# Delta-rule attention and two feed-forward stages: the corner blocks of the triangular inverses formed ahead, in two bursts of small matmuls a tile

## The chip, the cores and the metric

The kernel runs on one core of a Trainium2 chip. Its engines are TensorE (PE, matmuls; PEld, its weight loads), VectorE (DVE), ScalarE (ACT), GpSimd (POOL) and SyncE (SP), which here issues most DMAs. They run side by side, each in its own program order, and wait for one another on semaphores. The metric is the device time of one execution in microseconds (us), lower is better.

## The reference

For each of 32 heads (4 batches of 8) and 768 steps, with keys k normalised over their 48 dimensions:

```python
y[t] = q[t] @ state
v_old = state.T @ k[t]
state = state + beta[t] * outer(k[t], v[t] - v_old)
```

The results of the heads, laid side by side, are x (3072 tokens by 384). Two feed-forward stages follow:

```python
h = max(x @ w_in, 0);  x = (h * h) @ w_out              # d_ff 2048
g = x @ w_gate;        out = (silu(g) * (x @ w_val)) @ w_out2   # d_ff 1536
```

## The kernel before

**Chunks and tiles.** The 768 steps are cut into 12 chunks of 64, n = 0 to 11. Two chunks make a tile, t = 0 to 5 ("tiles two to six" are t = 1 to 5); chunk n is half s = n mod 2 of tile t = n // 2. Inside a chunk the recurrence is a triangular system: the 64x64 inverse has two 32x32 blocks on its diagonal and one block under it. The stages of a chunk on PE are: G (gram matrix of the keys), KS (keys times state, taken from v to give `resid`), QK, U (inverse times `resid`), Z (gram times the first half of U), DZ (second diagonal inverse times Z, taken off `u_tok`), Y (result), DS (state update), X (transposes, four a tile, by both chunks). Z and DZ stand in for the missing block under the diagonal. Each of these, X apart, is a burst of 32 small fp32 matmuls (64 for Y); the trace counts two instructions for one fp32 matmul, so x64 for 32.

**Inverses.** The diagonal blocks of the gram matrices go to `tri_scratch` in memory, and come back as `tri`, one 32x32 block in each of 128 partitions. "lane" (one ACT step, five on DVE) makes the scales from norms and beta; then `solve` inverts all 128 blocks by 31 column steps of two instructions. POOL does this for t = 1 to 5 (line 644). The result `tinv` goes out to `inv_scratch` and is loaded back as the blocks of `inv` by eight DMAs (`load_blocks`, line 415). U waits for them.

**The feed-forward work around it.** The first stage is seven units u = 0 to 6 (the first tile in two halves, 256 tokens wide; the rest 512 wide). Unit u has steps f = 0 to 17; PE does nine up matmuls for f < 16, and nine down matmuls for f - 2. Slot 2f lies between the up and the down matmuls of step f, slot 2f + 1 behind the down ones. `plan(u)` names for each slot the attention stages that go there, and PE, ACT and DVE all follow it. For f >= 1, ACT and DVE also make `h_hi` and `h_lo` of step f - 1, which the down matmuls read; an engine held up in a slot holds these back too. In units 2 to 5 the attention stages are those of tile t = u, in units 0 and 1 those of chunks 1 to 3. Unit 6 and the second feed-forward stage have no attention work.

**Banks.** The attention stages take two of three PSUM banks in turn, so a stage waits until the stage before it (one bank) and the one before that (the other) have been copied out.

**SP's queue** is written out by hand, in order: a DMA whose semaphore isn't there yet holds back all behind it. `k_sq` (line 469) is a load for the key norms. ACT squares it in the stage "sq", and "sq" of chunk 4 stands in slot 24 of unit 0, in ACT's order before an `h_hi`.

Of the kernel before, what the change touches and what calls it, by code (L numbers as in the profile page):

```python
# [5 lines left out]
def program(nc, kt, qt, kz, ky, vy, beta, w1, w2, out):  # L6
# [27 lines left out]
    inv_dram = nc.dram_tensor("inv_scratch", (NIT, P, HALF * HALF), f32, kind="Internal").ap()  # L34
    x1_dram = nc.dram_tensor("x1_scratch", (KC, P, NIT * T), f32, kind="Internal").ap()

    ctx = ExitStack()
    with ctx:
# [35 lines left out]
        gram = [sb(att_mem, f"gram{i}", [P, 2, 8, C]) for i in range(GRAMS)]  # L74
        qk = sb(att_mem, "qk", [P, 2, 8, C])
        inv = [sb(att_mem, f"inv{s}", [P, 16, C]) for s in range(2)]
# [66 lines left out]
        inv_stored = sem("inv_stored")  # L143
        first_stored = [sem(f"first_stored{i}") for i in range(3)]
# [61 lines left out]
        def plan(u):  # L206
# [11 lines left out]
            if u == 0:  # L218
# [22 lines left out]
                put(26, "QK", 2)  # L241
                put(27, "lane", 2)
                put(28, "U", 2)
                put(30, "Z", 2)
                put(31, "root", 4)
                put(32, "DZ", 2)
            elif u == 1:
                put(1, "Y", 2)
                put(3, "DS", 2)
                put(3, "scale", 3)  # L250
                put(5, "KS", 3)
                put(6, "QK", 3)
# [8 lines left out]
            else:  # L261
                t, p = u, u + 1
                n0, n1, p0, p1 = 2 * t, 2 * t + 1, 2 * p, 2 * p + 1
                if t < NIT:
                    if p < NIT:
                        put(0, "G", p0)
                        put(10, "G", p1)
                        put(16, "lane", p)
                    put(2, "sq", n1)
                    put(4, "root", n1)  # L270
                    put(8, "scale", n1)
                    chain(n0, dict(KS=2, QK=4, U=5, Z=7, DZ=9, Y=11, DS=12))
                    chain(n1, dict(KS=14, QK=15, U=17, Z=19, DZ=21, Y=23, DS=24))
# [15 lines left out]
        MATMULS = ("G", "QK", "KS", "U", "Z", "DZ", "Y", "DS", "X")  # L289
# [21 lines left out]
        def emptied(stage_):  # L311
# [8 lines left out]
            if name == "U":  # L320
                return [(ready, n + 1) for ready in u1_ready]
            if name == "Z":
                return [(ready, n + 1) for ready in z_ready]
# [52 lines left out]

        FILLED = {"G": g_filled, "U": u1_filled, "Z": z_filled, "Y": y_filled}
# [34 lines left out]
        def load_blocks(eng, t, s, i):  # L412
            for ab in range(2):
# [3 lines left out]
                              ).then_inc(inv_loaded[s], 16)  # L417

# [24 lines left out]
        def _(sp):  # L443
# [49 lines left out]
            def load_inverses(t, s):  # L493
                sp.wait_ge(inv_stored, 16 * t)
                sp.wait_ge(dz_filled, 2 * t + s - 1)
                for i in range(2):
                    load_blocks(sp, t, s, i)
# [41 lines left out]
            load_inverses(1, 0)  # L539
            load_inverses(1, 1)  # L540
# [3 lines left out]
            store_both(5)  # L544
            load_triangles(2)
# [7 lines left out]
            load_k(4)  # L553
            load_q(4)
            load_ktok(4)
            store_inverses(2)
            load_inverses(2, 0)
            load_inverses(2, 1)

            for u in range(2, NIT):  # L560
                t, p = u, u + 1
                n1, n2 = 2 * t + 1, 2 * t + 2
                if p < NIT:
                    load_prep(2 * p + 1)
                    store_both(2 * p)
# [5 lines left out]
                if p < NIT:  # L571
                    if p < NIT - 1:
                        load_prep(2 * p + 2)
                    store_both(2 * p + 1)
                load_q(n1)
                if n1 < NCH - 1:
                    load_ktok(n1)
# [577 lines left out]
```

## Time and profile before

| | us |
|---|---|
| median of 3 runs | 1049.47 |
| lowest and highest | 1049.29, 1050.03 |
| the profiled execution | 1047.97 |
| its span, first to last instruction | 1046.3 |

| engine | busy us | share of the span |
|---|---|---|
| PE | 990.5 | 95% |
| DVE | 408.2 | 39% |
| ACT | 303.0 | 29% |
| POOL | 208.1 | 20% |

The span is one execution as the hardware profiler saw it. The sums below are made against the 1047.97 us of that same execution; what lies outside its span is 1.7 us. The median of the runs is 1.5 us above it. A start time in the rows is counted from the start of the span.

### The profile page before, as it was taken

The numbers are of one execution on the slowest core, as the hardware profiler recorded it, in microseconds if no ns is written. First come the engines' busy times: TensorE is split into PE (matmuls) and PEld (weight loads), VectorE is DVE, ScalarE is ACT, GpSimd is POOL, SyncE is SP. The second block draws the span as 40 slices with busy tenths as digits, with TensorE's granted clock in tenths as the row PEclk, the third lists the DMA queues.
The fourth block names the chain that finished last, engine by engine and source line by source line (L and its number), as shares of the span: only waits on it lengthen the run. The fifth ranks groups of instructions, "written<-read, shape, count | busy, mean of one in ns | idle before, by whom it ended". The sixth has DMA issues, their size and how long they took to land.

```text
span 1046.3 us, 24211 instructions
## 1 busy us (share of the span) xinstructions
PE 990.5 (95%) x10752; PEld 823.0 (79%) x10752; DVE 408.2 (39%) x693; ACT 303.0 (29%) x599; POOL 208.1 (20%) x337
## 2 busy tenths in 40 slices
PE   2189999999999999999999999999999999999998
PEld 2178899788778878878888888888888888888887
DVE  3965644434434434543256521322312311322222
ACT  2225333333323333332245411221212211212121
POOL 1186381028307703820000000000000000000000
PEclk9999999999999999999999999999999999999999
DMA  7656423431452052130044010100100100100000
GB/s 232 189 151 197 143 74 86 131 95 53 110 154 63 26 152 80 52 107 23 2 173 145 15 61 1 50 11 1 61 1 1 61 1 1 61 1 0 31 1 31
DMA packets 74392, 73.88 MB, mean 71 GB/s; under 512 B 53168, under 2 KB 53296, under 8 KB 74288
## 3 DMA queue, kind: packets, MB, share of 16 engines
q1 hardware_dynamic: 68624, 64.99, 21.0%
q10 hardware_dynamic: 5664, 7.34, 2.2%
q8 instruction: 85, 1.39, 0.6%
q14 instruction: 19, 0.16, 0.1%
HBM read 56.59 MB, written 15.73 MB: 69 GB/s over the span
## 4 chain that ended last, share of the span: by engine, by line
PE 83%; POOL 8%; DVE 3%; DMA 3%; issue 1%; SPq 1%; ACT 0%; ACTq 0%; POOLq 0%; DVEq 0%
PE bank L895 82%; POOL tinv L399 4%; POOL prod L396 4%; DVE first_tinv L399 1%; DVE first_prod L396 1%; SPq L415 1%; DMA k_sq<-in_ky 1%; DMA inv_scratch<-tinv 1%; POOL tri L390 0%; DMA k_dim<-in_kt 0%; DMA tri_scratch<-gram 0%; DMA first_tri<-tri_scratch 0%; DVE h_lo L856 0%; PE bank L1024 0%; DMA inv<-inv_scratch 0%
## 5 line engine op out<-in xcount | busy, mean ns | idle before, releaser
L895 PE MATMUL bank<-x_hi,w_hi 128*128 128x512 f32 (+1 forms) x768 | 295.3, 384 | 1.2 <-DVE x_lo L831 1.2
L895 PE MATMUL bank<-x_lo,w_hi 128*128 128x512 f32 (+1 forms) x768 | 289.6, 377 | 0.0
L895 PE MATMUL bank<-x_hi,w_lo 128*128 128x512 f32 (+1 forms) x768 | 289.4, 377 | 0.0
L895 PE MATMUL bank<-h_hi,w_hi 128*128 128x512 f32 (+1 forms) x552 | 210.7, 382 | 2.6 <-DVE h_lo L856 2.5
L895 PE MATMUL bank<-h_hi,w_lo 128*128 128x512 f32 (+1 forms) x552 | 204.8, 371 | 0.0
L895 PE MATMUL bank<-h_lo,w_hi 128*128 128x512 f32 (+1 forms) x552 | 204.8, 371 | 0.0
L874 DVE TENSOR_TENSOR stage<-bank,stage 128x512 f32<-128x512 f32 x72 | 49.8, 692 | 318.5 <-ACT stage L741 318.5
L895 PEld LDWEIGHTS bank<-x_hi,w_hi 128*128 128x128 f32 x768 | 145.2, 189 | 29.4 <-DVE x_lo L831 1.6
L895 PEld LDWEIGHTS bank<-x_hi,w_lo 128*128 128x128 f32 x768 | 145.2, 189 | 26.5
L895 PEld LDWEIGHTS bank<-x_lo,w_hi 128*128 128x128 f32 x768 | 145.4, 189 | 24.9
L850 DVE TENSOR_TENSOR stage<-stage,bank 128x512 f32<-128x512 f32 (+1 forms) x112 | 68.4, 611 | 224.3 <-ACT stage L715 224.2
L741 ACT ACTIVATE stage<-bank 128x512 f32<-128x512 f32 x72 | 43.1, 598 | 329.7 <-PE bank L895 329.7
L715 ACT ACTIVATE stage<-bank 128x512 f32<-128x512 f32 (+1 forms) x112 | 60.0, 536 | 226.8 <-PE bank L895 218.7
L895 PEld LDWEIGHTS bank<-h_hi,w_hi 128*128 128x128 f32 x552 | 103.8, 188 | 26.6 <-DVE h_lo L856 5.6
L895 PEld LDWEIGHTS bank<-h_hi,w_lo 128*128 128x128 f32 x552 | 103.9, 188 | 18.1
L895 PEld LDWEIGHTS bank<-h_lo,w_hi 128*128 128x128 f32 x552 | 104.0, 188 | 16.8
L649 ACT ACTIVATE h_hi<-stage 128x512 fp32r<-128x512 f32 (+1 forms) x184 | 108.2, 588 | 6.9 <-PE bank L895 6.9
L399 POOL TENSOR_TENSOR tinv<-tinv,prod 128x31 f32<-128x31 f32 (+15 forms) x155 | 96.0, 619 | 12.1
L396 POOL TENSOR_TENSOR prod<-tri,tinv 128x31 f32<-128x31 f32 (+15 forms) x155 | 88.3, 570 | 12.2
L856 DVE TENSOR_TENSOR h_lo<-stage,h_hi 128x512 fp32r<-128x512 f32 (+1 forms) x112 | 76.3, 682 | 21.7 <-ACT h_hi L649 21.4
L390 POOL TENSOR_TENSOR tri<-tri,lane_nw 128x1024 f32<-128x1024 f32 x5 | 13.2, 2638 | 206.2 <-DVE lane_nw L795 206.2
L877 DVE TENSOR_TENSOR h_lo<-stage,h_hi 128x512 fp32r<-128x512 f32 x72 | 49.1, 682 | 5.1 <-ACT h_hi L649 5.1
(84 smaller groups left out, 576.6 us busy)
## 6 DMA issues: line engine op xcount, KB each, us to landing
w_raw<-in_w SPq DMA_DIRECT2D x12, 576.0 KB, 3.8
k_dim<-in_kt SPq DMA_DIRECT2D x12, 512.0 KB, 4.7
q_dim<-in_qt SPq DMA_DIRECT2D x12, 512.0 KB, 3.8
k_prep<-in_kt SPq DMA_DIRECT2D x10, 512.0 KB, 4.2
x1s<-in_w ACTq DMA_DIRECT2D x12, 384.0 KB, 4.7
k_sq<-in_ky SPq DMA_DIRECT2D x12, 384.0 KB, 3.7
v_tok<-in_vy SPq DMA_DIRECT2D x12, 384.0 KB, 4.0
x_scratch<-x1s SPq DMA_DIRECT2D x18, 256.0 KB, 3.1
```

Of the source, the lines that this page charges most:

```text
L390: then(eng.tensor_tensor(a[:, :, :], a[:, :, :], lane_nw[:, :].unsqueeze(1).to_broadcast([P, HALF, HALF]), ALU.mult))
L396: then(eng.tensor_tensor(share, a[:, j:j + 1, j + 1:HALF].to_broadcast(block), x[:, 0:j + 1, j:j + 1].to_broadcast(block), ALU.mult))
L399: then(eng.tensor_tensor(below, below, share, ALU.add))
L415: eng.dma_start(inv[s][ab * C + i * HALF:ab * C + (i + 1) * HALF, :, i * HALF:(i + 1) * HALF], inv_dram[t, at + ab:at + HALF:2, :].rearran ...
L649: return act.activation(dst, src, ACT.Copy)
L715: act.activation(stage[:, f % 2, 0:w], up_bank[f % 2][:, 0:w], ACT.Relu).then_inc(relu_done, 1)
L741: act.activation(stage[:, f % 2, :], gate_bank[f % 2][:, :], ACT.Silu).then_inc(silu_done, 1)
L850: dve.tensor_tensor(stage[:, f % 2, 0:w], stage[:, f % 2, 0:w], up_bank[f % 2][:, 0:w], ALU.mult).then_inc(square_done, 1)
L856: dve.tensor_tensor(h_lo[:, (f - 1) % 2, 0:w], stage[:, (f - 1) % 2, 0:w], h_hi[:, (f - 1) % 2, 0:w].bitcast(f32), ALU.subtract).then_inc( ...
L874: dve.tensor_tensor(slot, val_bank[f % 2][:, :], slot, ALU.mult).then_inc(hid_done, 1)
L877: dve.tensor_tensor(h_lo[:, (f - 1) % 2, :], stage[:, (f - 1) % 2, :], h_hi[:, (f - 1) % 2, :].bitcast(f32), ALU.subtract).then_inc(hid_lo ...
L895: return pe.matmul(dst, lhsT, rhs, start=start, stop=stop, **kw)
```

## The change

The inverse's block under the diagonal is now formed for tiles t = 1 to 5, by two bursts a tile on PE: N1 multiplies, for both chunks, the gram block with the first diagonal inverse, and N2 multiplies the second diagonal inverse with that, 64 matmuls of 32x32 with 32 columns in each. N1 is copied out (negated) into the free corner of the gram tile by two instructions on ACT and two on DVE, N2 into the free corner of `inv_both` by three on each. U then uses the full inverse, and Z and DZ are left out for chunks 2 to 11. N1 and N2 read the inverses from the gram tiles' unused corner; they are brought there by 12 new DMAs a tile (`load_cross`), 8 of which read a transposed copy, which POOL makes with one `tensor_copy` behind the solve and SP stores with two DMAs (`flip_scratch`). In the schedule G of a tile is taken two tiles ahead, in slots 9 and 14; "lane" moves to slot 1 of the unit before (slot 4 of unit 1 for t = 2, slot 6 of unit 2 for t = 3); N1 stands in slot 32 of the unit before (slot 26 of unit 0 for t = 1, slot 2 of unit 2 for t = 2), N2 in slot 4 of the tile's own unit (slot 28 of unit 0 for t = 1). SP's queue is rewritten to match.

```diff
@@ plan(u) @@
             if u == 0:
...
                 put(24, "sq", 4)
                 put(24, "KS", 2)
-                put(26, "QK", 2)
-                put(27, "lane", 2)
-                put(28, "U", 2)
-                put(30, "Z", 2)
+                put(26, "N1", 1)
+                put(28, "N2", 1)
+                put(30, "QK", 2)
                 put(31, "root", 4)
-                put(32, "DZ", 2)
+                put(32, "U", 2)
             elif u == 1:
                 put(1, "Y", 2)
                 put(3, "DS", 2)
                 put(3, "scale", 3)
+                put(4, "lane", 2)
                 put(5, "KS", 3)
                 put(6, "QK", 3)
                 put(8, "U", 3)
-                put(11, "Z", 3)
-                put(14, "DZ", 3)
-                put(16, "Y", 3)
-                put(18, "DS", 3)
+                put(10, "G", 6)
+                put(12, "Y", 3)
+                put(15, "DS", 3)
+                put(18, "G", 7)
...
                 if t < NIT:
+                    if t == 2:
+                        put(2, "N1", t)
                     if p < NIT:
-                        put(0, "G", p0)
-                        put(10, "G", p1)
-                        put(16, "lane", p)
+                        put(6 if t == 2 else 1, "lane", p)
+                        put(32, "N1", p)
+                    if t + 2 < NIT:
+                        put(9, "G", 2 * t + 4)
+                        put(14, "G", 2 * t + 5)
                     put(2, "sq", n1)
                     put(4, "root", n1)
+                    put(4, "N2", t)
                     put(8, "scale", n1)
-                    chain(n0, dict(KS=2, QK=4, U=5, Z=7, DZ=9, Y=11, DS=12))
-                    chain(n1, dict(KS=14, QK=15, U=17, Z=19, DZ=21, Y=23, DS=24))
+                    chain(n0, dict(KS=2, QK=5, U=7, Y=10, DS=12))
+                    chain(n1, dict(KS=15, QK=16, U=18, Y=21, DS=23))
@@ new copies out of PSUM and new loads @@
+        def take_whole(copy, stage_, ab):
...
+            for r in range(2):
+                copy(inv_both[early(ab), :, 12 * r:12 * r + 4, HALF:C], rows[0][:, :, r, :, :])
+            copy(inv_both[early(ab), :, 4:12, HALF:C], bank_rows(BANKS[stage_][1], ab)).then_inc(whole_ready[ab], 2)
...
+        def load_cross(eng, t, s):
+            block = gram[(2 * t + s) % GRAMS]
+            for bp in range(2):
+                at = lanes(s, 1) + bp * 16
+                eng.dma_start(block[bp * C + HALF:bp * C + C, :, :, HALF:C].rearrange("c r m i -> c (r m) i"),
+                              inv_dram[t, at:at + 16, :].rearrange("m (c i) -> c m i", i=HALF)
+                              ).then_inc(blocks_loaded[s], 16)
+            for x in range(2):
+                for r in range(2):
+                    at = lanes(s, 0) + (x ^ r) * 16 + 8 * r
+                    eng.dma_start(block[x * C:x * C + HALF, r, :, HALF:C],
+                                  flip_dram[t, at:at + 8, :].rearrange("m (i c) -> i m c", c=HALF)
+                                  ).then_inc(blocks_loaded[s], 16)
@@ SP, POOL, PE @@
             def load_triangles(t):
...
                     sp.wait_ge(sub_step, SUB * (t - 1))
+                    sp.wait_ge(flip_stored, 32 * (t - 1))
...
             def store_inverses(t):
...
+                sp.wait_ge(flipped, t)
+                for s in range(2):
+                    at = slice(lanes(s, 0), lanes(s, 0) + HALF)
+                    sp.dma_start(flip_dram[t, at, :], tri[at, :, :].rearrange("p s t -> p (s t)")
+                                 ).then_inc(flip_stored, 16)
...
             store_inverses(1)
             load_q(2)
-            load_inverses(1, 0)
-            load_inverses(1, 1)
+            load_inverses(1)
+            store_both(5)
+            load_triangles(2)
             load_prep(6)
             load_ktok(2)
             load_ky(4)
-            store_both(5)
-            load_triangles(2)
...
                 solve(pool, t, tri, tinv, prod, sub_step, SUB * (t - 1))
+                pool.tensor_copy(tri[:, :, :], tinv[:, :, :].rearrange("p c i -> p i c")).then_inc(flipped, 1)
...
+                elif name == "N1":
+                    for s in range(2):
+                        pe.wait_ge(blocks_loaded[s], 96 * n)
...
```

**SP, unit 0, from the storing of tile 1's inverses on.** `tri_scratch<-gram` are the stores of gram blocks, `k_sq<-in_ky` the load that ACT's "sq" reads. Before:

```order
L491 DMA inv_scratch<-tinv 128x1024
L459 DMA q_dim<-in_qt 128x1024
L415 DMA inv<-inv_scratch 32x16x32 x8
L447 DMA k_prep<-in_kt 128x1024
L464 DMA k_tok<-in_kz 128x768
L469 DMA k_sq<-in_ky 128x768
L407 DMA tri_scratch<-gram 32x16x32 x4
L487 DMA tri<-tri_scratch 128x1024
```

and now:

```order
L543 DMA inv_scratch<-tinv 128x1024
L547 DMA flip_scratch<-tri 32x1024 x2
L510 DMA q_dim<-in_qt 128x1024
L460 DMA gram<-inv_scratch 32x16x32 x2
L466 DMA gram<-flip_scratch 32x8x32 x4
L460 DMA gram<-inv_scratch 32x16x32 x2
L466 DMA gram<-flip_scratch 32x8x32 x4
L450 DMA inv_both<-inv_scratch 32x16x32 x8
L442 DMA tri_scratch<-gram 32x16x32 x4
L539 DMA tri<-tri_scratch 128x1024
L498 DMA k_prep<-in_kt 128x1024
L515 DMA k_tok<-in_kz 128x768
L520 DMA k_sq<-in_ky 128x768
```

Two stores and twelve loads are new ahead of the `k_sq` load, and the four gram stores with the `tri` load have moved from behind it to ahead of it.

**ACT, unit 0, steps 12 to 14.** `k_sq<-k_sq` is "sq" of chunk 4, in slot 24. Before:

```order
L715 ACTIVATE stage<-bank 128x256
L672 ACTIVATE k_sq<-k_sq 128x768
L649 ACTIVATE h_hi<-stage 128x256
L649 ACTIVATE w_hi<-x1s 128x768
L715 ACTIVATE stage<-bank 128x256
L649 ACTIVATE h_hi<-stage 128x256
L680 ACTIVATE lane_t<-tri 128x32
```

and now:

```order
L792 ACTIVATE stage<-bank 128x256
L749 ACTIVATE k_sq<-k_sq 128x768
L718 ACTIVATE h_hi<-stage 128x256
L718 ACTIVATE w_hi<-x1s 128x768
L792 ACTIVATE stage<-bank 128x256
L738 ACTIVATE gram<-bank 32x2x8x32 x2
L718 ACTIVATE h_hi<-stage 128x256
```

"sq" keeps its place; the copies of N1 are new behind it, and the lane step of tile 2 has left this stretch.

**PE, the beginning of unit 2, around slot 2** (`state,k_dim` is KS of chunk 4, `x_hi,w_hi` and the like are the up matmuls of the unit). Before:

```order
L895 MATMUL bank<-x_hi,w_lo 128x512
L895 MATMUL bank<-state,k_dim 64x48 x32
L895 MATMUL bank<-x_hi,w_hi 128x512
L895 MATMUL bank<-x_lo,w_hi 128x512
L895 MATMUL bank<-x_hi,w_lo 128x512
```

and now:

```order
L980 MATMUL bank<-x_hi,w_lo 128x512
L980 MATMUL bank<-gram 32x32 x64
L980 MATMUL bank<-state,k_dim 64x48 x32
L980 MATMUL bank<-x_hi,w_hi 128x512
L980 MATMUL bank<-x_lo,w_hi 128x512
```

N1 of tile 2 stands ahead of KS. The burst of G that stood one step earlier (slot 0) is gone from unit 2.

## Rows read from the trace of the kernel before

**Rows 1.** The page, the chain that ended last, by engine, as shares of the span

```profile
PE 83%; POOL 8%; DVE 3%; DMA 3%; issue 1%; SPq 1%; ACT 0%; ACTq 0%; POOLq 0%; DVEq 0%
```

**Rows 2.** Timeline of PE, unit 4: start us, duration us, engine, line, instruction

```profile
380.33 0.39 PE L895 MATMUL bank<-h_lo,w_hi 128*128 128x512 f32 x1
380.56 0.39 PE L895 MATMUL bank<-h_hi,w_lo 128*128 128x512 f32 x1
380.88 1.15 PE L895 MATMUL bank<-resid,inv 32*64 32x48 f32 x64
381.95 0.50 PE L895 MATMUL bank<-x_hi,w_hi 128*128 128x512 f32 x1
```

**Rows 3.** Timeline of PE, unit 4, around DS, whose weights have 48 columns

```profile
391.84 0.39 PE L895 MATMUL bank<-x_hi,w_lo 128*128 128x512 f32 x1
393.02 0.50 PE L895 MATMUL bank<-h_hi,w_hi 128*128 128x512 f32 x1
```

**Rows 4.** Timeline of PE around U of chunk 8, and at U of chunk 10

```profile
369.55 0.39 PE L895 MATMUL bank<-h_hi,w_lo 128*128 128x512 f32 x1
...
371.17 0.50 PE L895 MATMUL bank<-x_hi,w_hi 128*128 128x512 f32 x1
...
459.54 1.15 PE L895 MATMUL bank<-resid,inv 64*64 64x48 f32 x64 [0.77 <-DMA inv<-inv_scratch]
```

**Rows 5.** Timeline of the end of unit 3, ACT and DVE; a gram's two copies

```profile
353.89 0.62 ACT L649 ACTIVATE h_hi<-stage 128x512 fp32r<-128x512 f32 x1
...
361.03 1.08 ACT L649 ACTIVATE gram<-bank 128x512 f32<-128x512 f32 x2 [0.52 <-PE bank L895]
...
354.55 0.69 DVE L856 TENSOR_TENSOR h_lo<-stage,h_hi 128x512 fp32r<-128x512 f32 x1
```

**Rows 6.** Timeline of SP's queue, unit 0: start us, us spent issuing, DMA, count

```profile
96.36 0.34 SPq L491 DMA_DIRECT2D inv_scratch<-tinv  x1
...
99.28 6.10 SPq L415 DMA_DIRECT2D inv<-inv_scratch  x8
...
106.52 0.43 SPq L469 DMA_DIRECT2D k_sq<-in_ky  x1
107.05 2.93 SPq L407 DMA_DIRECT2D tri_scratch<-gram  x4
113.97 0.34 SPq L487 DMA_DIRECT2D tri<-tri_scratch  x1
```

**Rows 7.** Timeline of ACT, unit 0, slot 24; in brackets what it waited for

```profile
112.56 0.84 ACT L672 ACTIVATE k_sq<-k_sq 128x768 f32<-128x768 f32 x1 [2.39 <-DMA k_sq<-in_ky]
```

**Rows 8.** Timeline of PE, unit 0, the down matmuls behind slot 26

```profile
114.22 0.39 PE L895 MATMUL bank<-h_hi,w_hi 128*128 128x256 f32 x1 [0.20 <-DVE h_lo L856]
```

**Rows 9.** The DMAs that load the tile `inv` (line 415, 512 runs each)

```profile
DMA to landing us min/median/max: 1.9/2.4/5.1
```

**Rows 10.** Timeline of POOL, the solve of tile 2, first and last rows

```profile
119.06 2.38 POOL L390 TENSOR_TENSOR tri<-tri,lane_nw 128x1024 f32<-128x1024 f32 x1 [18.74 <-DVE lane_nw L795]
...
160.84 0.27 POOL L399 TENSOR_TENSOR tinv<-tinv,prod 128x31 f32<-128x31 f32 x1
164.01 0.96 POOL L642 MEMSET tinv<- 128x1024 f32 x1 [2.89 <-DMA inv_scratch<-tinv]
```

**Rows 11.** Timeline of DVE: first lane step of tile 2; squaring of step 2, unit 1

```profile
117.66 0.18 DVE L791 TENSOR_SCALAR lane_t<-lane_t 128x32 f32<-128x32 f32 x1 [0.36 <-ACT lane_t L680]
...
135.68 0.41 DVE L850 TENSOR_TENSOR stage<-stage,bank 128x256 f32<-128x256 f32 x1
```

**Rows 12.** Timeline of PE, unit 2, slot 2

```profile
182.98 1.15 PE L895 MATMUL bank<-state,k_dim 48*64 48x48 f32 x64
```

**Rows 13.** Timeline of PE, the first matmuls of unit 0

```profile
66.80 0.58 PE L895 MATMUL bank<-x_hi,w_hi 128*128 128x256 f32 x1 [1.17 <-DVE x_lo L831]
...
70.37 0.29 PE L895 MATMUL bank<-x_lo,w_hi 128*128 128x256 f32 x1
70.50 0.28 PE L895 MATMUL bank<-x_hi,w_lo 128*128 128x256 f32 x1
```

More of the change, by code:

```diff
@@ L73, in program @@
         q_dim = sb(att_mem, "q_dim", [P, 16, C])
-        gram = [sb(att_mem, f"gram{i}", [P, 2, 8, C]) for i in range(GRAMS)]
+        grams = [sb(att_mem, f"gram{i}", [P, 2, 2, 8, C]) for i in range(GRAMS // 2)]
+        gram = [grams[i // 2][:, i % 2, :, :, :] for i in range(GRAMS)]
         qk = sb(att_mem, "qk", [P, 2, 8, C])
-        inv = [sb(att_mem, f"inv{s}", [P, 16, C]) for s in range(2)]
+        inv_both = sb(att_mem, "inv_both", [P, 2, 16, C])
+        inv = [inv_both[:, s, :, :] for s in range(2)]
         tri = sb(att_mem, "tri", [P, HALF, HALF])
@@ L143, in program @@
         inv_stored = sem("inv_stored")
+        flipped = sem("flipped")
+        flip_stored = sem("flip_stored")
+        blocks_loaded = [sem(f"blocks_loaded{s}") for s in range(2)]
+        cross_filled = sem("cross_filled")
+        cross_ready = [sem(f"cross_ready{x}") for x in range(2)]
+        whole_filled = sem("whole_filled")
+        whole_ready = [sem(f"whole_ready{ab}") for ab in range(2)]
         first_stored = [sem(f"first_stored{i}") for i in range(3)]
@@ L321, in emptied @@
                 return [(ready, n + 1) for ready in u1_ready]
+            if name == "N1":
+                return [(ready, 2 * n) for ready in cross_ready]
+            if name == "N2":
+                return [(ready, 2 * n) for ready in whole_ready]
             if name == "Z":
@@ L577, in _ @@
                     load_ktok(n1)
+                if g < NIT:
+                    if g < NIT - 1:
+                        load_prep(2 * g + 2)
+                    store_both(2 * g + 1)
                 if p < NIT:
-                    load_triangles(p)
                     load_v(n2)
@@ L665, in run @@
                     store_triangles(act, n, 1)
+                elif name == "N1":
+                    act.wait_ge(cross_filled, n)
+                    for bp in range(2):
+                        act.activation(cross_rows(n, 0, bp), bank_rows(BANKS[stage_][bp], 0), ACT.Copy, scale=-1.0
+                                       ).then_inc(cross_ready[0], 1)
+                elif name == "N2":
+                    act.wait_ge(whole_filled, n)
+                    take_whole(copy, stage_, 0)
                 elif name == "fetch":
@@ L805, in run @@
                                           mask[:, :].unsqueeze(1).to_broadcast([P, 8, C]), ALU.mult).then_inc(qk_ready, 1)
+                elif name == "N2":
+                    dve.wait_ge(whole_filled, n)
+                    take_whole(copy, stage_, 1)
+                elif name == "N1":
+                    dve.wait_ge(cross_filled, n)
+                    for bp in range(2):
+                        dve.tensor_scalar(cross_rows(n, 1, bp), bank_rows(BANKS[stage_][bp], 1), -1.0, None, ALU.mult
+                                          ).then_inc(cross_ready[1], 1)
                 elif name == "KS":
@@ L901, in run, with u_whole @@
                 t, s = divmod(n, 2)
+                def u_whole():
+                    if t == 0:
+                        pe.wait_ge(u_ready, 2 * (n + 1))
+                    else:
+                        for ready in u1_ready:
+                            pe.wait_ge(ready, n + 1)
                 for one in sorted(BEFORE[stage_]):
@@ L938, in run @@
                     done.then_inc(ks_filled, 1)
+                elif name == "N1":
+                    for s in range(2):
+                        pe.wait_ge(blocks_loaded[s], 96 * n)
+                        block = gram[(2 * n + s) % GRAMS]
+                        for m in range(8):
+                            for r in range(2):
+                                for bp in range(2):
+                                    at = (8 * s + m) * HALF
+                                    done = mm(pair[bp][early(bp ^ r), at:at + HALF], block[late(bp), r, m, 0:HALF],
+                                              block[late(bp), r, m, HALF:C])
+                    done.then_inc(cross_filled, 1)
+                elif name == "N2":
+                    for ready in cross_ready:
+                        pe.wait_ge(ready, 2 * n)
+                    for s in range(2):
+                        block = gram[(2 * n + s) % GRAMS]
+                        for r in range(2):
+                            for a in range(4):
+                                for ab in range(2):
+                                    for x in range(2):
+                                        at = (8 * s + 4 * (x ^ r) + a) * HALF
+                                        done = mm(pair[x][early(ab), at:at + HALF], block[early(x), r, 2 * a + ab, HALF:C],
+                                                  block[early(x), r, 2 * a + ab, 0:HALF])
+                    done.then_inc(whole_filled, 1)
                 elif name == "U":
                     pe.wait_ge(inv_loaded[s], 64 * (t + 1))
+                    if t > 0:
+                        for ready in whole_ready:
+                            pe.wait_ge(ready, 2 * t)
                     if n == 0:
@@ L961, in run @@
                                     at = (4 * r + a) * D
-                                    done = mm(pair[bp][toks(ab), at:at + D], gram[n % GRAMS][early(bp), r, 2 * a + ab, :],
+                                    done = mm(pair[bp][late(ab), at:at + D],
+                                              gram[n % GRAMS][early(bp), r, 2 * a + ab, HALF:C],
                                               u_tok[early(bp), ab, 4 * r + a, :])
@@ L976, in run @@
                 elif name == "Y":
[L977 removed]
+                    u_whole()
                     pe.wait_ge(qk_ready, 2 * (n + 1))
```

52 lines of the change are left out of this document (33 added, 19 removed).

## The prediction, made before the changed kernel ran

> **What bounds the kernel now.** I read the chain that ended last first. PE has 83% of it and POOL 8% [rows 1], so the kernel is a stream of matmuls with a few places in which something else comes last. Next I read PE's timeline, to see what the small bursts take out of the stream, and then the queue of SP, ACT and POOL at the places where the chain leaves PE. There are two kinds of cost to tell apart. A burst displaces the big matmuls for as long as it runs. A wait costs what PE stands idle, and only where the waiting engine holds up a later matmul.
>
> In the steady part a 512-wide matmul starts every 0.23 us. Across a burst of 32 small matmuls the next start comes 1.39 us after the last one, so the burst takes 1.39 - 0.23 = 1.16 us [rows 2]. DS, whose weights are 48 columns wide and not 64, takes 393.02 - 391.84 - 0.23 = 0.95 us [rows 3]. PE waits hardly at all there: U of each tile's first chunk takes 1.39 us, 0.23 above the plain 1.16, since QK just before it must be copied out first; and U of chunk 10 waited 0.77 us for its inverse [rows 4].
>
> Unit 0 is different. ACT stood 2.39 us in slot 24, until the `k_sq` load had landed at 112.56 [rows 7]. That load was issued at 106.52, behind eight loads of inverses which in turn waited for the store issued at 96.36 [rows 6]. ACT's next instruction makes an `h_hi`, and 1.66 us after 112.56 PE goes on with the down matmuls that read it [rows 8]. So in the kernel before, SP's queue is already the last to arrive in this place, by a hair: anything put ahead of the `k_sq` load moves the end of the kernel.
>
> **The change, part by part.**
>
> Bursts taken out. Z and DZ go for ten chunks. Those of chunk 2 belong to unit 0 and are counted there; the 18 others are in the steady part: 18 x 1.16 = 20.9 us less.
>
> Bursts put in. N1 and N2 are 64 matmuls of 32x32 each, and the trace before has none of this shape. From 64 to 48 columns of weights a burst of 32 fell by 0.21 us, so at 32 columns it would be 0.74, and one of 64 matmuls at most 1.48. If 0.27 us of each burst is its start and end, and counted once, 1.2. If narrow weights gain nothing, 2 x 1.16 = 2.3. I take 1.45, near the slope of rows 2 and 3. For t = 2 to 5 that is 8 x 1.45 = 11.6 us more (9.6 to 18.6). The moved G bursts cost the same where they now stand: each slot has the up and the down matmuls of a step around it, and ACT's two copies of a gram (1.08 us, [rows 5]) are done within the nine matmuls (2.05 us) behind it.
>
> Waits that go. U now stands two slots behind QK, not one, which takes away 3 x 0.23 for chunks 4, 6 and 8; and the solve of tile 5 starts early in the unit, so the 0.77 goes too [rows 4]: 1.5 us less.
>
> The end of units 2, 3 and 4. N1 in slot 32 puts two copies on ACT, of the size of a gram's half, ahead of the last `h_hi`. After N1 ends: 1.08 for the copies, 0.62 for `h_hi`, 0.69 for `h_lo` [rows 5], together 2.4, while PE has nine down matmuls (2.05) before it needs that `h_lo`. About 0.4 us each, 3 x 0.4 = 1.2 us more (0 to 2.4).
>
> The steady part alone thus gains 20.9 + 1.5 - 11.6 - 1.2 = 9.6 us. N2's copies (three on each of ACT and DVE, some 1.5 us) hide behind the nine down matmuls in front of QK; were that cover gone they would cost up to 1.5 us a tile. SP, ACT and DVE otherwise have room. The work on PE is not where this change is decided.
>
> First wait, unit 0. The stage "sq" of chunk 4 still stands in slot 24. Ahead of its load SP now has: the wait for POOL's transposing copy, two stores, and the wait until they have landed. The copy has 1024 elements a partition, between a memset of 0.96 and a two-input multiply of 2.38 us of that size [rows 10]; I take 1.6. With the stores it starts the loads at about 101.2 and not 99.28: 1.9 us. Then twelve loads. The eight inverse loads took 6.10 us to issue [rows 6]; the twelve move as many 128-byte runs as eight did (4 of 512, 8 of 256). I take 5.5 us, of 3.8 to 9.1. Then the gram stores, the wait until they have landed, and the load of `tri`, which before stood behind: from 107.05 to 114.31 [rows 6], 7.3 us. The load itself took 6.0 us to land in heavy traffic; I take 5.0. Together 1.9 + 5.5 + 7.3 - 1.0 = 13.7 us later (8.7 to 20): ACT would stand in slot 24 for some 16 us. What is queued behind it is the `h_hi` of step 11 and everything after; PE gets through up matmuls 13 and N1, and then stands at the down matmuls of step 11 which started at 114.22 before [rows 8]. N1 of tile 1 is free, beneath that wait. The rest of unit 0 has N2, QK and U where it had U, Z and DZ: about 0.4 us less. So 13.3 us more. All else that this order delays (`k_tok`, `v_tok`) is needed later than it comes.
>
> Second wait, unit 2, slot 2. N1 of tile 2 waits for its blocks, and KS of chunk 4 and all of PE's stream stand behind it. The clock for both sides starts in unit 1, so the first wait shifts them alike; in times of the trace before: the square of step 2 ends at 136.1 [rows 11]; the five lane steps on DVE and POOL's start took 1.4 us (117.66 to 119.06, [rows 10, 11]): POOL begins at 137.5. A solve took 42.05 us (119.06 to 161.11, [rows 10]); this one runs later, beside wider work of DVE, so I take 43: 180.5. Copy 1.6, two stores and their landing 2.8, twelve loads 5.5, landing 2.2 (median 2.4, least 1.9, [rows 9]): 192.6, and the second half of N1 behind it 0.7: 193.3. Without a wait PE would reach N1 at 182.98 [rows 12] less the G burst that is gone from slot 0, 181.8, and end it at 183.3. The wait is 10.0 us (6 to 18). For tiles 3 to 5 there is none: from lane in slot 1 or 6 to N1 in slot 32 are 60 us and more against some 58, with tile 3, whose solve begins near slot 6 of unit 2, the nearest: its blocks come about 7 us early.
>
> The clock. After its long wait for the first inverse, PE began unit 0 with 17 matmuls from 66.80 to 70.37, one every 0.21 us, and from there on one starts every 0.12 to 0.13 [rows 13], although the granted clock is shown as 1.00 there; that is the step between 1.2 and 2.4 GHz, and those 17 at 0.21 in place of 0.12 cost 1.5 us. Both new waits are over 9 us long, and I charge each with that: 3.1 us (0 to 4). The Trainium skill (TensorE: Matmul & The Clock Gate, What's actually happening) says that an idle TensorE falls back to 1.2 GHz; rows 13 agree, and no row shows how a wait of 10 us in mid-stream fares.
>
> **Sum.** Against the profiled execution: 1047.97 - 9.6 + 13.3 + 10.0 + 3.1 = 1064.8. The median of the runs lies 1.5 us above that execution, so 1066.
>
> **The rivals.**
>
> One wait only. The second wait is the longer chain of estimates (solve, copy, loads). If tile 2's blocks come before PE does, 10.0 and 1.5 go: 1054.7. It needs a chain 10 us shorter than computed; the solve alone, which POOL does as before, is 42 of its 56. 0.08.
>
> Faster, by short exchange. The place is SP's queue in unit 0. If twelve loads and two stores are issued side by side with what is in flight, `k_sq` lands some 5.5 us late, not 13.7, and tile 2's blocks are there when N1 is reached. That gives 1047.97 - 9.6 + 5.1 + 1.5 + 1.5 = 1046.5. It decides for faster when both waits with their slow stretches come to less than 7.5 us. For it: one load alone takes 1.9 us at least to land [rows 9], and the 6.10 us for eight [rows 6] are a crowded stretch. Against it: 7.3 us of the delay were measured as they stand, in this queue. 0.08. As much gain from cheaper bursts is not to be had, since 8 bursts at 1.2 give only 2 us more.
>
> Dear bursts. The time of a small matmul may have a floor, so that 32 columns cost more than I think. In rows 2 an instruction takes 1.15 / 64 = 18 ns; at 25 ns N1 and N2 would be 3.2 us each, 14 us more in all: 1080. That is what a rule would give that the Trainium skill states (TensorE: Matmul & The Clock Gate, Wait — 56ns, not 53.3ns?): no start closer than about 25 ns to the last however few the columns. Rows 2 lie below it already, for bursts that alternate among four parts of the array, as N1 and N2 do. 0.04.
>
> **How the numbers follow.** Both waits and the gain as computed: 0.76, 1066, by itself 1056 to 1078. One wait: 0.08. Faster by short exchange: 0.08. Dear bursts: 0.04. In between, the waits short and the gain just eaten: 0.04. Lows of all terms together give 1048 - 13 + 8.3 + 6 + 1.5 = 1051, highs over 1085; the range 1053 to 1080 leaves out the fast case, the even case and the far tails, 2 in 10. The measurement tells 0.2% (2.1 us) from no change; so faster 0.08, same 0.04, slower 0.88.
>
> **What would show it.** In the profile after: ACT waiting in unit 0 for `k_sq` some 16 us instead of 2.39, with PE idle behind it for 12 or so; a row of PE in unit 2 with about 10 us of waiting for the `gram` loads ahead of a burst of 32x32; no Z and DZ from there on, bursts N1 and N2 of 1.2 to 1.5 us, and units 3 to 5 each shorter than before by roughly 2 us. The prediction is wrong if `k_sq` lands before 118 or tile 2's blocks come before PE needs them; its size is wrong first in the issue time of the twelve loads and in POOL's copy.

## The result, and the profile of the changed kernel

| | before | after |
|---|---|---|
| median of four runs, us | 1049.75 | 1070.7 |
| lowest and highest | 1049.29, 1050.25 | 1069.93, 1073.3 |
| the profiled execution | 1047.97 | 1070.59 |
| its span | 1046.3 | 1068.9 |

The changed kernel takes 1.0196 times as long (95% interval 1.018 to 1.0212). The prediction said 1066 (1053 to 1080).

First the page of the kernel after: the share of each engine in the chain that ended last, which answers to [rows 1], and the granted clock in 40 slices, which was 9 in each on the page of before.

```profile
PE 80%; POOL 8%; DVE 4%; DMA 3%; issue 2%; SPq 2%; ACT 1%; ACTq 0%; DVEq 0%; POOLq 0%
PEclk9679699799999999999999999999999999999999
```

PE's share fell by three points; DVE, SP's queue, ACT and "issue" (waits for nothing that the profile shows) rose by one each. The clock dips in slices 2, 3, 5 and 8. Slices 2 and 3 are not a difference between the kernels: there PE waits for the first inverses in both, and its bursts of 64 instructions take up to 1.99 us in both, where [rows 2] have 1.15, though the page of before shows 9. So that page doesn't show every slow stretch, and the rows' durations have to be read with it. New are slices 5 (106.9 to 133.6 us) and 8 (187 to 213.8 us). The list of PE's waits names both places (columns: total us, times, longest us):

```profile
PE bank L980 <- DVE h_lo L941: 16.9, 6, 13.2
PE bank L980 <- DMA gram<-flip_scratch: 9.8, 2, 6.5
PE bank L980 <- ACT inv_both L718: 2.1, 4, 0.6
PE bank L980 <- ACT gram L738: 1.5, 1, 1.5
```

Their rows on PE's and ACT's timelines (columns as in [rows 7] and [rows 8]):

```profile
125.59 0.84 ACT L749 ACTIVATE k_sq<-k_sq 128x768 f32<-128x768 f32 x1 [15.55 <-DMA k_sq<-in_ky]
127.25 0.58 PE L980 MATMUL bank<-h_hi,w_hi 128*128 128x256 f32 x1 [13.23 <-DVE h_lo L941]
205.62 1.08 PE L980 MATMUL bank<-gram 32*32 32x32 f32 x64 [6.54 <-DMA gram<-flip_scratch]
209.97 1.08 PE L980 MATMUL bank<-gram 32*32 32x32 f32 x64 [3.26 <-DMA gram<-flip_scratch]
212.50 1.96 PE L980 MATMUL bank<-state,k_dim 48*64 48x48 f32 x64 [1.46 <-ACT gram L738]
```

**First wait.** ACT stands 15.55 us for `k_sq` in slot 24 of unit 0 (2.39 before, [rows 7]). PE names DVE's `h_lo`, but DVE had waited for ACT's `h_hi`, and ACT for the load. PE's group begins at 127.25, where [rows 8] have 114.22: 13.03 us later. **Second wait.** In unit 2 both halves of N1 wait for their loads, 6.54 + 3.26 = 9.80 us, and KS behind them 1.46 more.

Where the 22.6 us (1068.9 - 1046.3) are, by the start of ACT's copy `x1s<-bank` at the end of each unit:

| unit | before | after | length before, after | change | the prediction's terms |
|---|---|---|---|---|---|
| 0 | 127.53 | 144.07 | | +16.54 | +14.8 |
| 1 | 177.66 | 195.01 | 50.13, 50.94 | +0.81 | 0 |
| 2 | 267.78 | 300.35 | 90.12, 105.34 | +15.22 | +11.4 |
| 3 | 357.87 | 388.82 | 90.09, 88.47 | -1.62 | -1.6 |
| 4 | 448.02 | 474.66 | 90.15, 85.84 | -4.31 | -3.9 |
| 5 | 535.02 | 557.62 | 87.00, 82.96 | -4.04 | -4.0 |

Behind unit 5 nothing differs (511.3 us in both). Units 3 to 5 gain what was worked out (9.97 us against 9.5); units 0 and 2 lose more than that, and unit 1 loses 0.8 where nothing was forecast.

SP's queue in unit 0, which answers to [rows 6]:

```profile
99.00 0.80 SPq L547 DMA_DIRECT2D flip_scratch<-tri  x2
101.92 0.85 SPq L460 DMA_DIRECT2D gram<-inv_scratch  x2
102.81 2.25 SPq L466 DMA_DIRECT2D gram<-flip_scratch  x4
109.36 4.35 SPq L450 DMA_DIRECT2D inv_both<-inv_scratch  x8
113.81 2.85 SPq L442 DMA_DIRECT2D tri_scratch<-gram  x4
118.10 0.34 SPq L539 DMA_DIRECT2D tri<-tri_scratch  x1
119.43 0.43 SPq L520 DMA_DIRECT2D k_sq<-in_ky  x1
```

The granted clock in stretches around the waits (columns: stretch, us, busy us of PE, PEld, DVE, ACT, POOL with their counts, granted clock, DMA share, GB/s):

```profile
127.00:136.00 9.00, 8.75 (x159) 8.47 (x160) 5.41 (x11) 3.79 (x10) 0.00 (x0) 0.50 0.01 2
136.00:144.00 8.00, 7.13 (x164) 6.50 (x164) 3.33 (x6) 2.08 (x6) 0.00 (x0) 0.97 0.40 116
205.00:218.50 13.50, 8.15 (x205) 6.58 (x205) 2.91 (x5) 2.31 (x4) 0.00 (x0) 0.51 0.77 181
218.50:222.00 3.50, 3.50 (x138) 2.76 (x137) 2.76 (x5) 1.80 (x6) 0.00 (x0) 1.00 0.12 36
```

After the first wait PE works for 9 us at the lower level (0.50, 1.2 GHz) before it has 2.4 GHz again.

### The profile page after: what moved, and what is told of

The parts are those of the page before. It is cut to its first block, busy times and chain, and to the rows that moved or that the text cites. A ratio compares the mean times of both kernels' runs of the same rounds, so it can differ in the third digit from the quotient of the medians.

```text
span 1068.9 us, 24285 instructions
## 1 busy us (share of the span) xinstructions
PE 984.3 (92%) x10752; PEld 819.8 (77%) x10752; DVE 413.4 (39%) x698; ACT 304.4 (28%) x604; POOL 215.7 (20%) x342
## 4 chain that ended last, share of the span: by engine, by line
PE 80%; POOL 8%; DVE 4%; DMA 3%; issue 2%; SPq 2%; ACT 1%; ACTq 0%; DVEq 0%; POOLq 0%
PE bank L980 79%; POOL tinv L434 4%; POOL prod L431 3%; DVE first_tinv L434 1%; DVE first_prod L431 1%; SPq L466 1%; DMA tri_scratch<-gram 1%; DMA k_sq<-in_ky 1%; DVE h_lo L941 1%; PE bank L1145 0%; DMA k_dim<-in_kt 0%; POOL tri L425 0%; SPq L460 0%; DMA flip_scratch<-tri 0%; DMA first_tri<-tri_scratch 0%
## 5 line engine op out<-in xcount | busy, mean ns | idle before, releaser
L434 POOL TENSOR_TENSOR tinv<-tinv,prod 128x31 f32<-128x31 f32 (+15 forms) x155 | 92.5, 597 | 12.1
```

The source lines that it names most:

```text
L434: then(eng.tensor_tensor(below, below, share, ALU.add))
```

## The experiments

The theory from here on: the steady gain is real, and the time is lost in two separate places, both in the order of SP's queue and both with a slow stretch of TensorE behind them. The rivals: the waits are one (take away the first, and the second grows), or the moved loads only pass the delay on.

**e1, the first wait alone.**

```diff
             load_q(2)
+            load_ky(4)
             load_inverses(1)
...
             load_ktok(2)
-            load_ky(4)
```

> The changed kernel with one line of SP's queue moved: the k_sq load of chunk 4 is issued before the twelve loads of tile 1's inverses, not behind them, the gram stores and the tri load. Theory (this load's place in the queue makes the first wait): ACT's wait in slot 24 falls from 15.6 us to under 2, PE's wait of 13.2 us behind it goes, and with it the stretch at half clock (3.6 us); the loads behind come about 3 us later, so N1 of tile 1 waits some 2 us instead. 1070.7 - 16.8 + 1.5 = about 1055 us; the wait in unit 2 stays at about 11 us. Rival (the exchange of the inverses as a whole is too long there, and N1, N2 or U of unit 0 wait in place of ACT): at least 1062.

1059.37 us, 1.0083 (1.0062 to 1.0104), between the theory's 1055 and the rival's 1062. ACT no longer waits, unit 0 ends at 135.99, and the second wait is as long as it was (6.50 + 2.94 + 1.46): the two are independent. But 11 us came back and not 15. One row of DVE, two of the queue and two of PE show the rest:

```profile
106.00 0.95 DVE L853 TENSOR_REDUCE norm<-k_sq 128x16 f32<-128x768 f32 x1
...
106.97 0.35 SPq L520 DMA_DIRECT2D k_sq<-in_ky  x1
107.42 2.08 SPq L460 DMA_DIRECT2D gram<-inv_scratch  x2
...
116.39 0.75 PE L980 MATMUL bank<-gram 32*32 32x32 f32 x64 [1.03 <-DMA gram<-flip_scratch]
123.28 0.37 PE L980 MATMUL bank<-h_hi,w_lo 128*128 128x256 f32 x1 [2.14 <-issue]
```

The `k_sq` load isn't free to go: its buffer is released by DVE's reduction of the chunk before, and the queue stands until 106.97. So the inverse loads start at 107.42 (101.92 in the kernel after), N1 waits 1.03 us, and N1 to U come late in unit 0. Then PE stands 2.14 us for nothing that the profile shows, and its granted clock is 0.50 from 124 to 132 us. How long that lasts isn't fixed: in e3, whose unit 0 has the same program, 15 matmuls of 256 columns are slow and not 24, and unit 0 ends 3.1 us earlier, at 132.85 (1 us of that is N1's wait, which isn't there).

**e4, the same cause in the kernel before.** Only `store_both(5)` and `load_triangles(2)` go ahead of the `k_prep`, `k_tok` and `k_sq` loads.

```diff
+            store_both(5)
+            load_triangles(2)
             load_prep(6)
             load_ktok(2)
             load_ky(4)
-            store_both(5)
-            load_triangles(2)
```

> The kernel before with only the order of SP's queue altered: the four gram stores and the tri load stand ahead of the k_prep, k_tok and k_sq loads, as in the changed kernel, with nothing else added. Theory: k_sq is issued some 7.1 us later (7.3 was my figure for this part of the delay), lands at about 119.6, and PE waits 7 us and then runs some microseconds at the slower clock: about 1059 us. Rival (the place was not critical, the wait is hidden): 1050.

1057.29 us, 1.0062 (1.0039 to 1.0085). The moved block by itself makes a wait of 7 of the 13 us, with nothing of N1 and N2 in the kernel:

```profile
121.19 0.58 PE L895 MATMUL bank<-h_hi,w_hi 128*128 128x256 f32 x1 [6.99 <-DVE h_lo L856]
120.00:124.00 4.00, 2.81 (x13) 2.81 (x14) 2.98 (x6) 2.14 (x6) 0.00 (x0) 0.50 0.03 10
```

A wait of 7 us is enough for the lower clock behind it, and shorter ones had it too (e1 above, e7 below). Unit 0 ends 8.6 us later.

**e2 and e3, the second wait alone, and both.** The attention stages of unit 2 go six slots later (N1 to slot 8). The grams of tile 4 stay in their slots, so that the first of them overwrites a gram tile before N2 has read it: the output isn't the reference's, the work is the same. SP stores and loads the inverses of tile 3 two loads earlier to suit (not shown).

```diff
+                    late = 6 if t == 2 else 0
                     if t == 2:
-                        put(2, "N1", t)
+                        put(2 + late, "N1", t)
...
-                    chain(n0, dict(KS=2, QK=5, U=7, Y=10, DS=12))
...
+                    chain(n0, dict(KS=2 + late, QK=5 + late, U=7 + late, Y=10 + late, DS=12 + late))
...
```

> The changed kernel with the attention stages of unit 2 (N1, KS, N2, QK, U, Y, DS of tile 2 and the scale step) six slots later, and the inverses of tile 3 stored and loaded two loads earlier in SP's queue to suit. Nothing is added or left out. Theory (N1 of tile 2 stands there too early for a solve that began in unit 1): its waits of 6.5 and 3.3 us, most of the 1.5 us of KS behind it and the slow clock after them (some 2.6 us) go: 1070.7 - 13 = about 1058, with the first wait unchanged. Rival (the lateness moves on to tile 3, whose solve starts in the same unit, or the later stages crowd the unit's end): 1064 or more.

1070.85 us, 1.0191 (1.0174 to 1.0207): no gain at all, as the rival had it. The wait is still 9.83 us, but it has another cause now:

```profile
215.37 0.26 ACT L762 ACTIVATE lane_t<-tri 128x32 f32<-128x32 f32 x1 [9.40 <-DMA tri<-tri_scratch]
220.46 1.96 PE L985 MATMUL bank<-state,k_dim 48*64 48x48 f32 x64 [9.83 <-DVE gram L894]
```

"lane" of tile 3 stands in slot 6 of this unit, and its load of `tri` is in SP's queue behind the 20 inverse loads of tile 2; the copies of N1, which free KS's bank, come only behind that step. In the kernel after, this hides beneath N1's wait. Both mended at once leave this one too:

> Both edits of the two runs before, together. Theory: the two waits are independent, so their prices add: 1070.7 - 16 - 13 = about 1042, below the kernel before (1049.7), since the steady part of the change gains 9 to 10 us. Rival (they share a cause, or the first hides part of the second): 1047 or more.

1058.2 us, 1.0067 (1.0049 to 1.0086), far from the theory's 1042, with 10.40 us of waiting in the same place (here too the gram is overwritten early).

**e5 and e6, the second wait and what hid behind it.** N1 of tile 2 in slot 8, its later stages and the grams of tile 4 behind, and the `tri` load of tile 3 ahead of the inverse loads (those of tile 3 two loads earlier, as in e2, not shown):

```diff
             store_inverses(2)
+            load_triangles(3)
             load_inverses(2)
-            load_triangles(3)
...
+                        put(16 if t == 2 else 9, "G", 2 * t + 4)
+                        put(20 if t == 2 else 14, "G", 2 * t + 5)
...
+                        chain(n0, dict(KS=9, QK=12, U=14, Y=17, DS=19))
+                        chain(n1, dict(KS=22, QK=23, U=25, Y=27, DS=29))
```

> The second wait again, after the run in which moving the stages of unit 2 left 9.8 us of waiting: there ACT and DVE stood in slot 6 for the lane step of tile 3, since the tri load stood behind the twenty loads of tile 2. Now the stages of tile 2 are six to seven slots later (KS one slot behind N1), the grams of tile 4 stand behind N2, and the tri load of tile 3 is issued ahead of the twenty loads. First wait left as it is. Theory (tile 2's exchange is late for everything that hangs on it, N1 and the tri load alike; both must be covered): unit 2 falls from 105.3 us to about 91, so 1070.7 - 14.5 = about 1056. Rival (the length of unit 2 comes from something else, or the crowded end of the unit gives it back): 1062 or more.

1056.2 us, 1.0055 (1.004 to 1.007). Unit 2 takes 90.25 us and not 105.34, no row waits for a gram load, and the first wait stays (13.79). With the `k_sq` load ahead as well:

> The same edit together with the k_sq load ahead of tile 1's exchange. Theory: prices add, 1059.4 - 14.5 = about 1045, faster than before by 0.4%. Rival (a shared cause): 1052 or more.

1043.69 us, 0.9933 (0.9919 to 0.9948): faster than the kernel before.

**e9, the last small wait.** After N2, QK waits for N2's copies:

```profile
222.52 1.16 PE L980 MATMUL bank<-q_dim,k_dim 48*64 48x64 f32 x64 [0.48 <-ACT inv_both L718]
310.41 1.10 ACT L718 ACTIVATE inv_both<-bank 32x256 f32<-32x256 f32 x3
310.29 1.36 DVE L837 COPY inv_both<-bank 32x256 f32<-32x256 f32 x3
```

e9 is e6 with QK, U, Y and DS of the first chunk one slot later in units 3 to 5.

```diff
-                        chain(n0, dict(KS=2, QK=5, U=7, Y=10, DS=12))
+                        chain(n0, dict(KS=2, QK=6, U=8, Y=11, DS=13))
```

> The kernel with the k_sq load first and tile 2 later, with QK, U, Y and DS of the first chunk of tiles 3 to 5 one slot further on, so that QK stands two groups of nine matmuls behind N2 and not one. Theory (QK waits 0.63, 0.63 and 0.34 us in that kernel's trace for the copies of N2, a wait that I had called hidden): 1.6 us less, 1043.7 to about 1042. Rival (the later stages wait instead): 1043.7 or more. The difference is near what a measurement can tell, so the waits in the trace decide.

1041.43 us (1039.24 to 1041.98), 0.9903 (0.9881 to 0.9925). The waits are gone, and units 3 to 5 take 87.77, 85.14 and 82.44 us (88.48, 85.87, 82.90 without this edit). It is the fastest version of the study.

**e7, the bursts for t = 2 to 5 only.** Units 0 and 1 are left as in the kernel before (with Z and DZ for tile 1's chunks) but for the two grams that go ahead. QK, U, Y and DS of each tile's first chunk are one slot later, as in e9.

```diff
-                put(26, "N1", 1)
-                put(28, "N2", 1)
-                put(30, "QK", 2)
+                put(26, "QK", 2)
+                put(27, "lane", 2)
+                put(28, "U", 2)
+                put(30, "Z", 2)
...
-                        put(2, "N1", t)
+                        put(0, "N1", t)
```

> The new blocks only for tiles 2 to 5 (t counted from 0); tile 1 keeps Z and DZ, its unit 0 and SP's order there are those of the kernel before, so the solve of tile 2 starts there as before and its blocks are in place before unit 2. N1 of tile 2 in slot 0 of unit 2, QK of a tile's first chunk one slot further from N2. Theory (the bursts are worth their price, only the two exchanges of the early tiles are late): bursts 16 x 1.16 off, 8 x 1.3 on, the U waits 1.5 off, 1.2 on at the unit ends: 1049.7 - 8.5 = about 1041 us, unit 0 as before at 127.5 us, no row of PE waiting for gram loads. Rival (the new bursts, copies and loads cost elsewhere what they save): 1048 or more.

1043.66 us, 0.994 (0.9923 to 0.9956). Tile 2's blocks come in time even for slot 0 of unit 2, since "lane" of tile 2 stands in slot 27 of unit 0 here. The median is 2.7 us above what was expected. The trace is of the fastest of the four executions (1040.69), so it can't show where the others lost that. What it does show is a unit 0 that ends 1.9 us later than before (129.43): SP's queue is 2.8 us later at the `k_sq` load (109.30 against 106.52, [rows 6]), ACT stands 4.45 us, PE 2.25 us, and the clock reads 0.62 for the 4 us behind that.

**e10 and e11, the reordering alone, and in e7.** The kernel before with the `k_sq` load first, and e7 with the same edit:

```diff
+            load_ky(4)
             load_inverses(1, 0)
             load_inverses(1, 1)
...
-            load_ky(4)
```

> The kernel before, with one edit: the load of chunk 4's k_sq goes ahead of the eight inverse loads of tile 1, so that ACT no longer stands in slot 24 of unit 0. It asks how much of the best version's gain is this reordering alone and has nothing to do with N1 and N2. Theory (the gain is mainly the bursts taken out): ACT's 2.39 us wait goes, PE gains at most the 1.7 us for which it stood behind it, and U of chunk 2 gets its inverse about 0.5 us later: 1048.5 us, within 0.2% of the kernel before. Rival (the queue's order was the whole gain): 1042 or less.

> The version in which only tiles three to six are changed (units 0 and 1 as before but for two grams), plus the load of k_sq ahead of the inverse loads. In that version ACT stood 4.45 us for k_sq in unit 0, and the granted clock went to 0.62 for the 4 us behind it; unit 0 ended at 129.43. If that wait is what is left of unit 0's loss, unit 0 ends near 127.5 and the time is 1041 to 1041.5 us, even with the best version (1041.4). Rival: the inverse loads behind it come late for U of chunk 2 and give it back: 1043.5, as without the edit.

1059.16 us, 1.0075 (1.0054 to 1.0096), and 1048.03 us, 0.997 (0.9958 to 0.9982). Both theories and both rivals missed. The same edit that gave 11 us after the change costs 8.6 before it (e10):

```profile
106.97 0.33 SPq L469 DMA_DIRECT2D k_sq<-in_ky  x1
107.41 5.03 SPq L415 DMA_DIRECT2D inv<-inv_scratch  x8
113.54 2.15 SPq L407 DMA_DIRECT2D tri_scratch<-gram  x4
121.19 0.34 SPq L487 DMA_DIRECT2D tri<-tri_scratch  x1
...
124.41 0.26 ACT L680 ACTIVATE lane_t<-tri 128x32 f32<-128x32 f32 x1 [9.03 <-DMA tri<-tri_scratch]
```

The load waits in the queue for DVE's reduction, all behind it moves back, and the `tri` load, issued at 113.97 in [rows 6], goes out at 121.19. "lane" of tile 2 stands in slot 27 of unit 0 in both versions, and ACT waits there for the load, 9.03 us and 8.81 us. Two things differ in the changed kernel, where the same edit pays: "lane" is in slot 4 of unit 1, and the wait that the edit takes away is 15.55 us and not 2.39. No run separates them. So the gain of the fastest version is not that of the reordering alone.

**e8, the price of the clock.** The kernel after with N1 of tile 1 run ten times, so that PE has work through most of the first wait.

```diff
-                    for s in range(2):
+                    for s in [0, 1] * (10 if n == 1 else 1):
                         pe.wait_ge(blocks_loaded[s], 96 * n)
```

> The changed kernel, in which PE runs the N1 burst of tile 1 ten times in place of once (each writes the same values), so that it is busy through nearly all of the 13 us in which ACT waits for the k_sq load. The wait itself stays. Theory (the slow stretch behind the first wait, 127.3 to 136.4 us at a granted clock of 0.50, comes from PE standing idle before it): the clock stays at 1.00 and the 3.6 us it cost come back: about 1067. Rival (small 32x32 matmuls don't count as work for the clock, or the clock falls for another reason): 1070.7, the same granted clock behind the wait as before. Rival 2 (the copies behind a longer burst come late): 1073.

1093.59 us, 1.0399 (1.0373 to 1.0424): every expectation missed, since the filling itself outlasted the wait.

```profile
117.52 1.50 PE L980 MATMUL bank<-gram 32*32 32x32 f32 x128 [2.20 <-issue]
137.53 1.93 PE L980 MATMUL bank<-gram 32*32 32x32 f32 x128 [1.52 <-issue]
140.00:144.00 4.00, 1.93 (x128) 1.79 (x128) 0.00 (x0) 0.00 (x0) 0.00 (x0) 0.50 0.01 4
```

A repeat takes at least 1.93 + 1.52 = 3.45 us, nearly half of it a wait for nothing shown. The clock reads 1.00 up to 117 us and 0.50 from 120 on, although PE never stood longer than 3.44 us. So this run doesn't say what the wait would cost with the clock kept up. That question is open; what the slow stretches cost is read from rows, below.

## Why the prediction was right, and where its terms were off

**Bound and mechanism: right.** The change is decided in SP's queue, at the two places named: `k_sq` in slot 24 of unit 0 (e1, e4) and tile 2's blocks in unit 2 (e5).

**The steady gain: right, 1 us too small.** In e9, where no long wait is left and QK stands a slot later, units 1 to 5 together are 10.7 us shorter than before by the traces (396.81 against 407.49); 9.6 were forecast, and the bursts are cheaper than that by 8 x 0.15 = 1.2. Unit 0 is still 4.1 us longer.

**The first wait: 13.03 us, forecast 13.7 (13.3 with the 0.4 that the bursts of unit 0 were to give back), by errors that cancel: luck in the size.** The `k_sq` load was issued at 119.43, 12.91 us after [rows 6] have it. Of these, 2.64 are the later start of the loads (1.9 forecast: POOL's copy took 2.02 us, not 1.6, and the solve ended 0.6 later), 5.75 are the longer row of loads (11.89 us against 6.14; 5.5 forecast), and 4.5 the moved block (7.3 forecast: the gram stores landed 1.4 us after the last was issued, and not 4.0). The load then took 6.16 us and not 5.0 (6.04 before).

**The second wait: 9.8 us, forecast 10.0.** The chain was right in its links:

```profile
153.70 2.52 POOL L425 TENSOR_TENSOR tri<-tri,lane_nw 128x1024 f32<-128x1024 f32 x1 [52.22 <-DVE lane_nw L872]
196.20 2.10 POOL L713 COPY tri<-tinv 128x1024 f32<-128x1024 f32 x1
```

The solve took 42.5 us (43), the copy 2.10 (1.6). From POOL's start to the last landing it was 56.3 us where 55.1 were forecast, and PE came to N1 1.1 us later after that start than forecast, so the two errors cancel. What the prediction hadn't is the 1.46 of KS: it stands in the same slot as N1 and waits until a bank that N1 filled has been copied out. Before, this slot had nothing ahead of KS.

**The clock: mis-sized.** It was charged with 1.5 us a wait, from 17 slow matmuls [rows 13]. After the first wait the stretch at 0.50 lasts 9 us. From the waiting group to the end of unit 0 are 144.07 - 127.25 = 16.82 us; before, 127.53 - 114.22 = 13.31. That is 3.5 more, where the prediction had 1.5 - 0.4 = 1.1; the exchange of bursts is in it. The rows give the slow stretch by itself: 32 matmuls of 256 columns start 0.21 us apart in place of 0.12, and N2 takes 1.93 us and not 1.29, together 3.6. After the second, KS takes 1.96 us (1.15 in [rows 12]), and nine matmuls of 512 columns start every 0.43 us and not 0.23: 0.8 + 9 x 0.20 = 2.6 us. Together that is 3.5 us above the terms of the sum, the largest miss of it; the forecast lies 4.7 us below the time. There is no fixed price to take in its stead. Behind a wait of 2.3 us for nothing shown, at the same place of the same unit 0, e6 had 24 slow matmuls and e9 had 13:

```profile
120.00:124.00 4.00, 3.79 (x27) 3.56 (x29) 0.00 (x0) 0.18 (x1) 0.00 (x0) 0.50 0.50 149
124.00:128.00 4.00, 4.00 (x79) 3.66 (x76) 2.65 (x5) 0.51 (x2) 0.00 (x0) 0.50 0.92 329
...
120.00:124.00 4.00, 2.64 (x13) 2.64 (x13) 0.45 (x2) 0.08 (x1) 0.00 (x0) 0.62 0.44 74
124.00:128.00 4.00, 3.70 (x119) 3.32 (x121) 2.53 (x5) 0.69 (x2) 0.00 (x0) 0.96 0.87 297
```

The first two rows are of e6, the others of e9.

**N1 and N2: right in kind, 1.45 forecast.**

```profile
307.67 1.29 PE L980 MATMUL bank<-gram 32*32 32x32 f32 x128
```

The row's 1.29 us are 10 ns an instruction, or 20 ns a matmul of two instructions. The Trainium skill (TensorE: Matmul & The Clock Gate, Wait — 56ns, not 53.3ns?) states that no matmul starts closer than about 25 ns to the last; for these bursts, which alternate among parts of the array, the rows show otherwise, and the rival of dear bursts is out.

**A cover that wasn't there.** The prediction called N2's copies hidden by the nine down matmuls ahead of QK. They are not quite: 0.34 to 0.63 us a tile, 2.1 in all. The copies take 1.10 and 1.36 us, but they begin only once N2 has ended and the work ahead of them on ACT and DVE is done. e9 against e6 takes the waits away and gains 0.71 + 0.73 + 0.46 = 1.9 us in units 3 to 5.

**The balance.** The profiled execution is 5.8 us longer than the sum's 1064.8: 3.5 for the clock, 2.1 for N2's copies, 1.5 for KS and 0.8 for unit 1, less 0.7 and 0.2 for the two waits and 1.2 for cheaper bursts. That closes it to within about 1 us, since N1's two halves at the lower clock in unit 2 are not in it.

**The rivals.** "One wait only" and "faster by short exchange" ask for blocks or a `k_sq` load that come in time: in this kernel neither does. In the mended versions both do, and there the time is 1041 to 1044, near the 1046.5 of the second. It was right on how thin the margin is, and wrong on what would close it: the place of two loads and six slots, not faster DMAs.

## What to carry to other kernels

Before a step is moved in a hand-written queue, write down for each entry both when its data is wanted and when its semaphore comes: the `k_sq` load that was too late behind the inverse loads made them 5.5 us later in e1 and 8.1 in e10 when put ahead (about 1 of it was there before that load). When one wait is taken away, look at once for the next entry of the same queue, here the `tri` load, the next to be late in e2 and in e10. And charge a long wait of TensorE with more than its length: the slow stretch behind it cost here about 1.6 us after 7.0 us of waiting, 2.6 after 9.8 and 3.5 after 13.2, each from one trace, with other small changes in it. This is a size and no rule, since waits of 2.0 to 2.4 us in e1, e3, e6, e7 and e9 had 11 to 24 slow matmuls behind them.

## What the runs showed of the hardware that was not expected

- The clock after a wait in mid-stream: it reads 0.50 in the stretch in which e4's wait of 7 us ended, and for 9 us behind the wait of 13.2 us. It comes back at once: matmuls of 256 columns start 0.21 us apart up to 136.40 and 0.12 apart from 136.54 on.
- PE stands at times for nothing that the profile shows, in the middle of a group of down matmuls. In the six versions with the `k_sq` load first it does so in unit 0, between 117 and 124 us: 2.14 (e1), 2.04 (e3), 2.35 (e6), 2.31 (e9), 1.00 (e10) and 0.67 us (e11). Others do so later: 0.74 in unit 0 of e5, 1.51 in unit 2 of e2. No row says why, and it isn't explained here. Of e9:

```profile
121.36 0.37 PE L990 MATMUL bank<-h_hi,w_lo 128*128 128x256 f32 x1 [2.31 <-issue]
```

- A long run of bursts of 32x32 matmuls is slower than its parts: one burst of 128 instructions takes 1.29 us in the steady part. With ten in a row (e8) one starts every 3.45 us at best, at the lower clock; the first gap, 2.20 us, falls in a stretch that reads 1.00. What holds them back isn't shown.
- POOL's copy that transposes 32x32 blocks in each partition (128x1024, fp32) took 2.02 to 2.10 us, between a memset (0.96) and a two-input multiply (2.52).
